# Attention stage: another order of work on PE, VectorE and ScalarE, and three small matrix products in another shape

## The chip, the cores and the metric

The kernel runs on one core of one Trainium2 chip. The metric is the device time of one execution in microseconds (us); lower is better. The profile is of one such execution. PE is TensorE (PEld its weight loads), DVE is VectorE, ACT is ScalarE, POOL is GpSimd, SP issues most of the transfers. A difference of about 0.3% is what the measurement can tell from none.

## The reference, cut to what matters

Pooled attention (8 batches, 8 heads, 576 tokens, 64 columns), a soft mixture of experts whose dispatch weights are a softmax over all tokens, and a dense layer with a gated norm.

```python
k_p = k.reshape(B, H, S // 8, 8, D).mean(axis=3)      # 72 pooled keys
v_p = v.reshape(B, H, S // 8, 8, D).mean(axis=3)
attn = softmax(q @ k_p.T / sqrt(D))                   # 576 x 72 for each head
x = (attn @ v_p) as [B*S, 512]
logits = x @ phi                                      # 32 slots
d = exp(logits - logits.max(0)) / sum over tokens     # dispatch
slot_input = d.T @ x
# ... 8 experts, then c @ slot_out, then the dense layer
```

## The kernel before

The first stage takes the 8 batches one after another. A batch has 5 tiles of tokens: four of 128 tokens and one of 64 (tile 4, in which two groups of heads lie side by side). A batch is written as 5 steps, `t` = 1 to 5, and a step works on several tiles at once: the scores of tile `t + 2`, the sums of tile `t + 1`, the transposes of tile `t`, the logits of tile `t - 1`. Tiles 5, 6 and 7 of a batch are tiles 0, 1 and 2 of the next. Below, 0', 1' and 2' are those tiles of the next batch. The order on each engine is written out by hand, in one `step` function for each engine; batches 1 to 6 run in a loop whose body holds two batches, batch 0 and the end have their own code. There is no scheduler: what is queued behind a wait on its engine waits too.

The path of a tile: `scores` on PE (L1313, tile 4 L1309) writes two PSUM banks of which there is one set. DVE takes the row maximum (L960, `smax`) and subtracts it (L966, into `attn`); only when that is done may `scores` of the next tile start. ACT takes `exps` (L665). DVE sums (L973) and takes the reciprocal (L978), POOL multiplies (L533, `norm`). PE transposes the tile (`aT_t`, L1356, tile 4 L1352), ACT copies the transposes out (`aT_evac`, L641), PE multiplies them by `vphi` (`lt_t`, L1380, tile 4 L1375), ACT copies (`lt_evac`), PE folds the four column groups (`l_t`, L1387), DVE copies the logits (`logit_evac`, L985).

Once a batch:
- `vphi` is pooled v times phi. PE makes `wphi` (`wphi_t`, L1323), ACT copies it out (`wphi_evac`, four copies), PE transposes it (`vphi_t`, L1330 to L1332: three of 128 columns, one of 32 rows, one of 64 rows), DVE copies and folds it (`vphi_evac`, L989 to L991). `lt_t` of tile 0 waits for it.
- the slot maximum of the batch: DVE `lmax_tokens` (L997), PE `lmax_t` (L1396), DVE `new_max` (L1002, then L1006 against the running maximum), PE `mb_t` (L1402, which spreads 32 numbers over 128 partitions with a product over 32 rows), DVE `d_sub` (L1012), ACT `d_exp` (L697, L701), PE `dat_t` (L1416), ACT `dat_evac`, PE `datT_t` (L1425), ACT `datT_evac`, PE `slot_t` (L1434), DVE `slot_acc` (L1022).
- POOL also pools k and v (L374, L378). SP loads k, v and q two batches ahead and an expert's weights in each batch.

`lt_t` has five blocks of the contraction (four of 128 rows, one of 76) and four column groups of 32: blocks 0 to 3 run beside each other in the four groups, block 4 follows alone in group 0.

## Time and profile before

| | us |
|---|---|
| runs shown, median | 441.24 |
| lowest, highest of 3 | 440.08, 441.43 |
| the profiled execution | 440.7 |
| its span | 438.9 |
| scores of batch 1's tile 3 begin | 38.27 |
| the same point of batch 7 | 145.50 |
| first product of the experts | 165.98 |
| dense layer from about | 212 |

Between 38.27 and 145.50 lie six like batches, 17.87 us each. PE's granted clock is full from 19 us on. Of the span PE is busy 94%, DVE 70%, POOL 56%, ACT 54%. A busy PE includes modelled ends of instructions; the distance from one start to the next tells what it really spends. The last 227 us are the dense layer, where PE is busy 221.75 us.

### The profile page before, as it was taken

The page shows a single profiled execution, that of the slowest core. Times are in us where ns is not written, and L with a number is a line of the kernel's source. Part 1 is how long each engine was busy: PE and PEld are TensorE (multiplying, and loading weights), DVE is VectorE, ACT ScalarE, POOL GpSimd, SP SyncE. Part 2 cuts the span into 40 slices and gives each one's busy share as a digit, 9 for nine tenths or more (in the row PEclk, how much of TensorE's full clock was granted, in tenths as well). Part 3 has the DMA queues.
Part 4 walks back from the last instruction along what each step waited for, and adds up shares of the span by engine and source line. Part 5 has one row for each costly group of instructions (what it writes and reads, how often), then busy time and mean ns, then how long its engine had stood idle before and what let it go on. Part 6 is the DMA issues. An engine that isn't in the chain of part 4 may idle for free.

```text
span 438.9 us, 9468 instructions
## 1 busy us (share of the span) xinstructions
PE 413.2 (94%) x3303; PEld 319.1 (73%) x3303; DVE 307.3 (70%) x543; ACT 238.8 (54%) x497; POOL 243.8 (56%) x346
## 2 busy tenths in 40 slices
PE   6788989899899889999899999999999999999997
PEld 6666777677777664455687887888888888888886
DVE  4878788787887747355889976777777777777211
ACT  1457775667756542153777655656555656555310
POOL 2579988888883311020143375757677666676540
PEclk8999999999999999999999999999999999999999
DMA  8847789769695699996001676677666666766732
GB/s 322 331 126 307 309 326 390 288 246 419 247 433 191 231 397 346 431 424 284 1 7 43 131 143 117 130 141 139 134 133 114 135 132 134 143 135 115 157 73 48
DMA packets 79212, 91.68 MB, mean 209 GB/s; under 512 B 67024, under 2 KB 67408, under 8 KB 74448
## 3 DMA queue, kind: packets, MB, share of 16 engines
q1 hardware_dynamic: 74016, 82.07, 60.9%
q10 hardware_dynamic: 5168, 9.24, 6.3%
q8 instruction: 16, 0.26, 0.2%
q14 instruction: 12, 0.10, 0.1%
HBM read 66.13 MB, written 9.44 MB: 172 GB/s over the span
## 4 chain that ended last, share of the span: by engine, by line
PE 75%; DVE 12%; ACT 5%; issue 4%; POOL 3%; DMA 1%; ACTq 0%; DVEq 0%
PE banks L1697 14%; PE banks L1698 14%; PE banks L1699 14%; PE banks L1313 5%; PE banks L1560 3%; PE banks L1669 3%; PE banks L1582 3%; PE banks L1356 2%; PE banks L1416 2%; DVE smax L960 2%; DVE attn L966 2%; DVE ssum L973 2%; PE banks L1387 2%; PE banks L1380 2%; ACT aT L641 1%
## 5 line engine op out<-in xcount | busy, mean ns | idle before, releaser
L1697 PE MATMUL banks<-wo_hi,uh 128*128 128x512 f32 x280 | 110.5, 395 | 0.1
L1698 PE MATMUL banks<-wo_lo,uh 128*128 128x512 f32 x280 | 110.0, 393 | 0.0
L1699 PE MATMUL banks<-wo_hi,ul 128*128 128x512 f32 x280 | 109.1, 390 | 0.0
L609 POOL TENSOR_TENSOR ul<-u_col,uh 128x1024 fp32r<-128x1024 f32 x30 | 71.9, 2397 | 18.6 <-ACT uh L641 18.2
L876 ACT ACTIVATE sq<-u,st 128x1024 f32<-128x1024 f32 x36 | 41.5, 1152 | 39.9 <-DVE u L1198 39.9
L533 POOL TENSOR_TENSOR attn<-attn,srec 128x576 f32<-128x576 f32 (+1 forms) x40 | 43.1, 1078 | 35.5 <-DVE srec L978 35.5
L1697 PEld LDWEIGHTS banks<-wo_hi,uh 128*128 128x128 f32 x280 | 52.6, 188 | 12.7 <-DVE ul L1215 0.5
L1699 PEld LDWEIGHTS banks<-wo_hi,ul 128*128 128x128 f32 x280 | 52.5, 188 | 12.1
L1698 PEld LDWEIGHTS banks<-wo_lo,uh 128*128 128x128 f32 x280 | 52.6, 188 | 11.3
L1198 DVE SCALAR_TENSOR_TENSOR u<-banks,ex 128x1024 f32<-128x1024 f32 x35 | 42.7, 1223 | 24.5 <-ACT ex L867 24.4
L1188 DVE TENSOR_REDUCE st<-banks 128x1 f32<-128x1024 f32 x35 | 42.6, 1216 | 18.3 <-PE banks L1669 18.3
L867 ACT ACTIVATE ex<-banks,st 128x1024 f32<-128x1024 f32 x35 | 39.0, 1115 | 18.4 <-DVE st L1188 17.7
L641 ACT ACTIVATE uh<-u_col 128x1024 fp32r<-128x1024 f32 x30 | 31.7, 1058 | 30.2 <-DMA u_col<-u_blk 16.3
L1313 PE MATMUL banks<-kblk,qb 128*128 128x144 f32 x256 | 40.6, 303 | 5.3 <-DVE attn L966 2.4
L1313 PEld LDWEIGHTS banks<-kblk,qb 128*128 128x128 f32 x256 | 34.0, 194 | 10.1 <-DVE attn L966 4.7
L1229 DVE TENSOR_SCALAR osb<-banks,rs 128x512 f32<-128x512 f32 x35 | 25.9, 741 | 19.5 <-PE banks L1699 19.5
L665 ACT ACTIVATE attn<-attn 128x576 f32<-128x576 f32 (+1 forms) x40 | 25.4, 636 | 25.5 <-DVE attn L966 25.1
L1208 DVE STREAM_TRANSPOSE u_blk<-u 128x1024 f32<-128x1024 f32 x30 | 37.4, 1246 | 1.9
L595 POOL TENSOR_SCALAR st<-st 128x1 f32<-128x1 f32 x36 | 6.9, 191 | 52.5 <-ACT sq L876 52.2
L374 POOL TENSOR_TENSOR vraw<-vraw 128x1152 f32<-128x1152 f32 (+1 forms) x14 | 29.5, 2108 | 7.4 <-DMA vraw<-in_v 7.4
L960 DVE TENSOR_REDUCE smax<-banks 128x8 f32<-128x576 f32 (+1 forms) x40 | 27.2, 680 | 8.4 <-PE banks L1313 8.4
L973 DVE TENSOR_REDUCE ssum<-attn 128x8 f32<-128x584 f32 (+1 forms) x40 | 27.8, 694 | 6.7 <-ACT attn L665 6.4
(179 smaller groups left out, 692.0 us busy)
## 6 DMA issues: line engine op xcount, KB each, us to landing
...
```

The lines of the kernel that those rows point to most:

```text
L533: pool.tensor_tensor(a, a, per_head(srec[bit(tile)], t)[:, :, :, None].to_broadcast([P, tile_pairs(t), 2, SP]), ALU.mult) \
L609: pool.tensor_tensor(ul[par][:, :, :].rearrange("p c (q t) -> p (c q) t", q=4), v, uh[par][:, :, :].bitcast(F32).rearrange("p c (q t) -> p ...
L867: act.activation(ex[par][:, :, :], h_banks(par), ACT.Exp, bias=st[k % STATS]["nmax"][:, :], accum_out=st[k % STATS]["den"][:, :]).then_inc ...
L876: act.activation(sq[par][:, :], u[k % URING][:, :], ACT.Square, scale=-float(FF), bias=st[k % STATS]["usum"][:, :], accum_out=st[k % STATS ...
L973: dve.tensor_reduce(per_head(ssum[par], t), head_sums(tile[1], t), AX.X, ALU.add).then_inc(sem("ssum"), 1)
L1188: dve.tensor_reduce(st[k % STATS]["nmax"][:, :], h_banks(k % 2), AX.XY, ALU.max, negate=True).then_inc(sem("nmax"), 1)
L1198: dve.scalar_tensor_tensor(u[k % URING][:, :].rearrange("p (a n) -> p a n", a=2), h_banks(par), 1.0, ex[par][:, :, :], ALU.mult, ALU.mult, ...
L1208: dve.transpose(u_blk[slot][:, :, :, k % 2, :].rearrange("p c q t -> p (c q) t"), u[k % URING][:, :].rearrange("p (b f) -> p b f", f=BLK)) \
L1313: last = pe.matmul(s_view[:, j, 0:2 * SP], q_cols(par, t, j), kblk[par][:, j, :], start=True, stop=True)
L1697: pe.matmul(ps[4 + par], uh[par][:, c, :], wo_hi[:, c, :], start=(c == 0), stop=False)
L1698: pe.matmul(ps[4 + par], uh[par][:, c, :], wo_lo[:, c, :], start=False, stop=False)
L1699: last = pe.matmul(ps[4 + par], ul[par][:, c, :], wo_hi[:, c, :], start=False, stop=(c == FC - 1))
```

## The change

It has two parts.

*Shapes.* `vphi_t` becomes four transposes of 128 rows; `wphi` is 512 columns wide, and its last 76 columns lie in partitions where the fourth block leaves room, so ACT copies five pieces. In `lt_t` the fifth block, of 76 rows, is no longer one product of 128 columns in group 0 but four of 32 columns, one in each group (tile 4: four of 32 columns in place of two of 64). `mb_t` takes all 128 rows; DVE's running maximum becomes a `tensor_scalar` with the old maximum as a pointer scalar.

*Order.* On PE, DVE and ACT the steps of batches 1 to 7 are written out anew. POOL and SP keep their order. Batch 0 keeps its order but for `vphi_evac` of batch 1, which stands at its end; `lmax_tokens` and the last `logit_evac` of a batch move into step 1 of the next.

```diff
-        wphi = bump("wphi", [P, PAIRS * PAIR])
+        wphi = bump("wphi", [P, 4 * P])
...
                 for j in range(PAIRS):
-                    g = 32 * GROUP[j]
-                    last = copy(wphi[g:g + 32, PAIR * j:PAIR * (j + 1)], b_head[g:g + 32, 0:PAIR])
-                last.then_inc(sem("wphi_sb"), 1)
+                    g, n = 32 * GROUP[j], min(PAIR, 4 * P - PAIR * j)
+                    copy(wphi[g:g + 32, PAIR * j:PAIR * j + n], b_head[g:g + 32, 0:n])
+                copy(wphi[LAST_ROWS, 0:BLOCKS[4]], b_head[LAST_ROWS, PAIR - BLOCKS[4]:PAIR]).then_inc(sem("wphi_sb"), 1)
...
+                elif t == 1:
+                    aT_evac(ahead(b, par, 0), 0)
+                    aT_evac(ahead(b, par, 0), 1)
+                    lt_evac(ahead(b, par, 0))
+                    aT_evac(ahead(b, par, 1), 0)
+                    aT_evac(ahead(b, par, 1), 1)
+                    if not last:
+                        kblk_fill(b + 1, 1 - par, 0)
+                    exps(ahead(b, par, 3))
+                    if last:
+                        v72_evac(b, par)
+                    else:
+                        kblk_fill(b + 1, 1 - par, 1)
+                elif t == 2:
+                    lt_evac(ahead(b, par, 1))
+                    exps(ahead(b, par, 4))
+                    aT_evac(ahead(b, par, 2), 0)
+                    d_exp(b - 1, (False,))
+                    v72_evac(b, par)
+                    aT_evac(ahead(b, par, 2), 1)
+                    vpad_fill(b + 1, 1 - par)
+                elif t == 3:
+                    lt_evac(ahead(b, par, 2))
+                    d_exp(b - 1, (True,))
+                    exps(ahead(b, par, 5))
+                    aT_evac(ahead(b, par, 3), 0)
+                    aT_evac(ahead(b, par, 3), 1)
                     alpha_exp(b - 1, 1 - par)
+                    dat_evac(b - 1)
+                elif t == 4:
+                    lt_evac(ahead(b, par, 3))
+                    aT_evac(ahead(b, par, 4), 0)
+                    aT_evac(ahead(b, par, 4), 1)
+                    exps(ahead(b, par, 6))
+                    datT_evac(b - 1)
+                    wphi_evac(b + 1)
+                else:
+                    lt_evac(ahead(b, par, 4))
+                    exps(ahead(b, par, 7))
...
-                dve.tensor_tensor(slot_max[par][:, :], lmax_new[:, :], slot_max[1 - par][:, :], ALU.max).then_inc(sem("m_ready"), 1)
+                dve.tensor_scalar(slot_max[par][:, :], lmax_new[:, :], slot_max[1 - par][:, :], None, ALU.max).then_inc(sem("m_ready"), 1)
...
+                    logit_evac(ahead(b, par, -1))
+                    tile_sums(ahead(b, par, 2))
+                    lmax_tokens(b - 1)
+                    tile_max(ahead(b, par, 3))
+                    tile_rec(ahead(b, par, 2))
+                    tile_sub(ahead(b, par, 3))
+                    batch_max(b - 1)
+                    logit_evac(ahead(b, par, 0))
+                    running_max(b - 1, 1 - par)
+                elif t == 2:
+                    sub_max(ahead(b, par, 4))
+                    d_sub(b - 1)
+                    tile_sums(ahead(b, par, 3))
+                    tile_rec(ahead(b, par, 3))
+                    logit_evac(ahead(b, par, 1))
+                    tile_sums(ahead(b, par, 4))
+                elif t == 3:
+                    tile_max(ahead(b, par, 5))
+                    tile_rec(ahead(b, par, 4))
+                    tile_sub(ahead(b, par, 5), dat_count(b - 1, 0))
+                    tile_sums(ahead(b, par, 5))
+                    logit_evac(ahead(b, par, 2))
+                    tile_rec(ahead(b, par, 5))
+                elif t == 4:
+                    tile_max(ahead(b, par, 6))
                     den_acc(b - 1, 1 - par)
-                if not (last and t + 2 >= TILES) and not (first and t in (1, 3)):
-                    sub_max(ahead(b, par, t + 2), None if t != 3 or first else dat_count(b - 1, 0))
-                if not first:
-                    if t == 1:
-                        new_max(b - 1, 1 - par)
-                    if t == 2:
-                        d_sub(b - 1)
-                    if t == 5:
-                        slot_acc(b - 1, 1 - par)
-                logit_evac(ahead(b, par, t - 1))
-                if t == 5:
-                    lmax_tokens(b)
+                    tile_sub(ahead(b, par, 6))
+                    logit_evac(ahead(b, par, 3))
+                    tile_sums(ahead(b, par, 6))
+                else:
+                    tile_max(ahead(b, par, 7))
+                    tile_rec(ahead(b, par, 6))
+                    tile_sub(ahead(b, par, 7))
+                    slot_acc(b - 1, 1 - par)
+                    vphi_evac(b + 1, 1 - par)
...
-                for n in range(1, 4):
-                    pe.transpose(b_head[:, 32 + P * (n - 1):32 + P * n], wphi[:, P * n:P * (n + 1)], ident[:, :])
-                pe.transpose(b_head[:, 0:32], wphi[0:32, 0:P], ident[0:32, 0:32])
-                pe.transpose(b_head[0:BLOCKS[4], 32 + 3 * P:96 + 3 * P], wphi[0:64, 4 * P:4 * P + BLOCKS[4]], ident[0:64, 0:64]).then_inc(sem("vphi_ps"), 1)
+                for n in range(4):
+                    last = pe.transpose(b_head[:, P * n:P * (n + 1)], wphi[:, P * n:P * (n + 1)], ident[:, :])
+                last.then_inc(sem("vphi_ps"), 1)
...
-                    for k, m in enumerate(BLOCKS):
-                        g = k % 4
-                        last = pe.matmul(b_lt[32 * g:32 * (g + 1), 0:P], vphi[par][0:m, k, :], aT[bit(tile)][0:m, k, :],
-                                         start=(k < 4), stop=(k + 4 >= NB), tile_position=(0, 32 * g))
+                    for k in range(4):
+                        pe.matmul(b_lt[32 * k:32 * (k + 1), 0:P], vphi[par][:, k, :], aT[bit(tile)][:, k, :],
+                                  start=True, stop=False, tile_position=(0, 32 * k))
+                    for g in range(4):
+                        r = slice(32 * g, 32 * (g + 1))
+                        last = pe.matmul(b_lt[r, r], vphi[par][0:m, NB - 1, :], aT[bit(tile)][0:m, NB - 1, r], start=False, stop=True, tile_position=(0, 32 * g))
...
-                pe.matmul(bank[:, 0:SLOTS], slot_max[par][0:SLOTS, :].to_broadcast([SLOTS, P]), ident[0:SLOTS, 0:SLOTS], start=True, stop=True).then_inc(sem("mb_ps"), 1)
+                pe.matmul(bank[:, 0:SLOTS], slot_max[par][:, :].to_broadcast([P, P]), ident[:, 0:SLOTS], start=True, stop=True).then_inc(sem("mb_ps"), 1)
...
+                    scores(ahead(b, par, 3))
+                    lt_t(ahead(b, par, 0))
+                    aT_t(ahead(b, par, 1))
+                    l_t(ahead(b, par, 0))
+                    lmax_t(b - 1, 1 - par)
+                elif t == 2:
+                    scores(ahead(b, par, 4))
+                    lt_t(ahead(b, par, 1))
+                    mb_t(b - 1, 1 - par)
+                    aT_t(ahead(b, par, 2))
+                    l_t(ahead(b, par, 1))
+                elif t == 3:
+                    scores(ahead(b, par, 5))
+                    dat_t(b - 1, 1 - par, (0, 1))
+                    lt_t(ahead(b, par, 2))
+                    dat_t(b - 1, 1 - par, (2, 3))
+                    l_t(ahead(b, par, 2))
+                    aT_t(ahead(b, par, 3))
+                elif t == 4:
+                    scores(ahead(b, par, 6))
+                    dat_t(b - 1, 1 - par, (4,))
+                    lt_t(ahead(b, par, 3))
+                    aT_t(ahead(b, par, 4))
+                    datT_t(b - 1)
+                    wphi_t(b + 1)
+                    l_t(ahead(b, par, 3))
+                else:
+                    scores(ahead(b, par, 7))
+                    slot_t(b - 1, 1 - par)
+                    v72_t(b + 1, 1 - par)
+                    lt_t(ahead(b, par, 4))
+                    vphi_t(b + 1)
+                    l_t(ahead(b, par, 4))
+                    aT_t(ahead(b, par, 5))
```

DVE, from the end of step 5 into step 1 of the loop's second batch. `smax` is the maximum, `attn` the subtraction, `ssum` and `srec` sum and reciprocal, `c_all` a tile's logits, `lmax_new` and `slot_max` the slot maximum. Before:

```order
L966 TENSOR_TENSOR attn<-banks,smax_86 128x4x2x72
L1022 SCALAR_TENSOR_TENSOR acc_slot<-acc_slot,alpha_94,banks 128x128
L985 ISA
L985 COPY c_all<-banks 128x32
L997 TENSOR_REDUCE lmax<-c_all 128x32
L988 REGISTER_ALU
L989 COPY vphi_80<-banks 128x32
L990 TENSOR_REDUCE vphi_80<-banks 128x96
L991 COPY vphi_80<-banks 76x32
L973 TENSOR_REDUCE ssum_88<-attn 128x8
L978 RECIPROCAL srec_90<-ssum_88 128x8
L959 REGISTER_ALU
```

and after:

```order
L989 TENSOR_TENSOR attn<-banks,smax_86 128x4x2x72
L1054 SCALAR_TENSOR_TENSOR acc_slot<-acc_slot,alpha_94,banks 128x128
L1019 REGISTER_ALU
L1020 COPY vphi_80<-banks 128x32
L1021 TENSOR_REDUCE vphi_80<-banks 128x96
L1022 COPY vphi_80<-banks 76x32
L1016 ISA
L1016 COPY c_all<-banks 128x32
L998 TENSOR_REDUCE ssum_88<-attn 128x8
L1028 TENSOR_REDUCE lmax<-c_all 128x32
L981 REGISTER_ALU
L982 TENSOR_REDUCE smax_87<-banks 128x8
```

`vphi_evac` has moved ahead of the logits of the old batch, `lmax` behind the sums of tile 2, and the reciprocal of tile 2 behind the maximum of tile 3.

ACT, step 1 of the same batch (`aT` the transposes, `lt` the product's copy, `attn` the exponential). Before:

```order
L641 ACTIVATE lt_68<-banks 128x128
L664 REGISTER_ALU
L665 ACTIVATE attn<-attn 128x4x2x72
L675 ISA
L641 ACTIVATE aT_79<-banks 128x512
L675 REGISTER_ALU
L641 ACTIVATE aT_79<-banks 76x128
L641 ACTIVATE kblk_75<-kp 64x4x72
```

and after:

```order
L642 ACTIVATE lt_68<-banks 128x128
L676 ISA
L642 ACTIVATE aT_79<-banks 128x512
L676 REGISTER_ALU
L642 ACTIVATE aT_79<-banks 76x128
L646 REGISTER_ALU
L642 ACTIVATE kblk_75<-kp 64x4x72
L665 REGISTER_ALU
L666 ACTIVATE attn<-attn 128x4x2x72
```

The exponential of tile 3 stands behind the copies of tile 1's transposes, no longer ahead of them.

PE, step 5 of the loop's first batch (L1313/L1377 scores of 2', L1434/L1503 `slot_t`, L1375/L1438 and L1442 `lt_t` of tile 4, L1356/L1419 `aT_t` of 0', L1387/L1456 `l_t`, L1340/L1403 `v72_t`, L1330/L1394 `vphi_t`). Before:

```order
L1313 MATMUL banks<-kblk_67,qb_62 128x144 x4
L1434 MATMUL banks<-v_0_82,datT 32x64 x8
L1364 ISA
L1375 MATMUL banks<-aT_79,vphi_81 32x64 x6
L1356 MATMUL banks<-ident,attn 128x128 x4
L1356 MATMUL banks<-ident,attn 76x128
L1387 MATMUL banks<-fold_50,lt_69 128x32
L1340 MATMUL banks<-ident,vT_76 72x128 x4
L1330 MATMUL banks<-ident,wphi 128x128 x3
L1331 MATMUL banks<-ident,wphi 128x32
L1332 MATMUL banks<-ident,wphi 76x64
```

and after:

```order
L1377 MATMUL banks<-kblk_67,qb_62 128x144 x4
L1503 MATMUL banks<-v_0_82,datT 32x64 x8
L1403 MATMUL banks<-ident,vT_76 72x128 x4
L1427 ISA
L1438 MATMUL banks<-aT_79,vphi_81 32x64 x4
L1442 MATMUL banks<-aT_79,vphi_81 32x32 x4
L1394 MATMUL banks<-ident,wphi 128x128 x4
L1456 MATMUL banks<-fold_50,lt_69 128x32
L1419 MATMUL banks<-ident,attn 128x128 x4
L1419 MATMUL banks<-ident,attn 76x128
```

`v72_t` and `vphi_t` have moved up, `l_t` of tile 4 and `aT_t` of tile 0' to the end.

## Rows read from the trace of the kernel before

**Rows 1.** Busy time by engine in one batch: stretch, length, busy (instructions), clock, DMA.
```profile
73.75:91.78 18.03, 16.64 (x214) 13.10 (x213) 14.53 (x34) 12.12 (x36) 14.77 (x12) 1.00 0.82 321
```

**Rows 2.** Waits of two batches (73.75 to 109.61): total us, times, longest.
```profile
PE banks L1380 <- ACT aT L641: 1.3, 2, 0.7
...
PEld banks L1387 <- ACT lt L641: 1.3, 6, 0.3
```

**Rows 3.** Timeline, scores of tile 3 in batches 1 and 7: start, length, what.
```profile
38.27 1.25 PE L1313 MATMUL banks<-kblk,qb 128*128 128x144 f32 x8
...
145.50 1.25 PE L1313 MATMUL banks<-kblk,qb 128*128 128x144 f32 x8
```

**Rows 4.** Timeline of PE over batch 3, without weight loads.
```profile
73.76 1.25 PE L1313 MATMUL banks<-kblk,qb 128*128 128x144 f32 x8
74.94 0.42 PE L1396 MATMUL banks<-ident,lmax 128*32 128x128 f32 x8
75.18 0.60 PE L1380 MATMUL banks<-aT,vphi 128*32 128x128 f32 x10
...
77.11 0.71 PE L1309 MATMUL banks<-kblk,qb 128*64 128x144 f32 x8 [0.49 <-DVE attn L966]
78.47 0.63 PE L1380 MATMUL banks<-aT,vphi 128*32 128x128 f32 x10 [0.65 <-ACT aT L641]
79.03 0.40 PE L1402 MATMUL banks<-ident,slot_max 32*128 32x32 f32 x2
79.36 0.77 PE L1356 MATMUL banks<-ident,attn 128*128 128x128 f32 x5
...
80.50 1.24 PE L1313 MATMUL banks<-kblk,qb 128*128 128x144 f32 x8 [0.22 <-issue]
...
84.67 1.25 PE L1313 MATMUL banks<-kblk,qb 128*128 128x144 f32 x8
...
87.79 1.25 PE L1313 MATMUL banks<-kblk,qb 128*128 128x144 f32 x8
88.98 0.43 PE L1434 MATMUL banks<-v,datT 72*32 72x64 f32 x16
89.25 0.42 PE L1375 MATMUL banks<-aT,vphi 128*32 128x64 f32 x12
...
90.57 0.61 PE L1340 MATMUL banks<-ident,vT 128*72 128x128 f32 x4
91.01 0.49 PE L1330 MATMUL banks<-ident,wphi 128*128 128x128 f32 x3
...
91.79 1.25 PE L1313 MATMUL banks<-kblk,qb 128*128 128x144 f32 x8
```

**Rows 5.** Timeline of DVE, POOL and ACT in step 1 of the same batch.
```profile
75.52 0.74 DVE L960 TENSOR_REDUCE smax<-banks 128x8 f32<-128x576 f32 x1
...
76.30 0.76 DVE L966 TENSOR_TENSOR attn<-banks,smax 128x576 f32<-128x576 f32 x1
...
76.79 1.41 POOL L374 TENSOR_TENSOR vraw<-vraw 128x576 f32<-128x576 f32 x1
...
77.09 0.68 ACT L665 ACTIVATE attn<-attn 128x576 f32<-128x576 f32 x1 [1.00 <-DVE attn L966]
...
77.29 0.93 DVE L1006 TENSOR_TENSOR slot_max<-lmax_new,slot_max 128x1 f32<-128x1 f32 x1
77.68 0.74 ACT L641 ACTIVATE aT<-banks 128x512 f32<-128x512 f32 x2
```

**Rows 6.** One line, all its instructions: ns min/median/max; then a row of the timeline.
```profile
L1006 DVE TENSOR_TENSOR slot_max<-lmax_new,slot_max x8: 158/929/942, 41.8 to 159.2; 128x1 f32<-128x1 f32 x8
...
90.62 0.34 DVE L1022 SCALAR_TENSOR_TENSOR acc_slot<-acc_slot,alpha,banks 128x128 f32<-128x128 f32 x1
```

**Rows 7.** Groups of two batches: busy us, mean ns of one.
```profile
L641 ACT ACTIVATE wphi<-banks 32x147 f32<-32x147 f32 x8 | 2.2, 280 | 0.1
```

**Rows 8.** Busy time from the end of the attention stage into the experts, columns as in rows 1.
```profile
146.00:206.00 60.00, 56.91 (x716) 31.16 (x714) 33.98 (x78) 22.57 (x53) 9.85 (x16) 1.00 0.97 385
```

181 lines of the change are left out of this document (84 added, 97 removed).

## The prediction, made before the changed kernel had run

> **What bounds the kernel now.** I read the table of busy time by stretch first. In a batch of the loop no engine but PE is near its limit: of 18.03 us PE is busy 16.64, POOL 14.77, DVE 14.53, ACT 12.12 [rows 1]. POOL and DVE are close enough behind that PE can't fall far before one of them takes over. The loop takes (145.50 - 38.27) / 6 = 17.87 us a batch [rows 3], all of it at PE's full clock.
>
> Then the waits and the timeline of PE. Twice in each batch PE stands still on the tile chain: 0.49 us before the scores of tile 4, which wait for DVE's subtraction of tile 3, and 0.65 us before `lt_t` of tile 1, which waits for ACT's copy of the transposes [rows 2, 4]. Three times `l_t` waits for ACT's `lt_evac`, 1.3 us in six waits of two batches, so 0.22 each [rows 2]. And 0.22 us before the scores of 0' is issue [rows 4]. That is 0.49 + 0.65 + 3 x 0.22 + 0.22 = 2.0 us of standing still in a batch, and 16.0 us of work.
>
> The scores have one set of banks, so a second limit is the chain scores, maximum, subtraction: 1.25 + 0.74 + 0.76 = 2.75 us and some hand-over for each full tile [rows 4, 5]. Four of these and a short one are near 13 us: not the bound by itself, but it decides wherever DVE or PE starts its part late.
>
> **The change, part by part.** I cut a batch at the starts of scores on PE: 3 to 4 is 77.11 - 73.76 = 3.35 us, 4 to 0' is 80.50 - 77.11 = 3.39, 0' to 2' is 87.79 - 80.50 = 7.29, 2' to the next 3 is 91.79 - 87.79 = 4.00, together 18.03 [rows 4].
>
> *Price of the new `lt_t`.* Now its start and the next start are 79.03 - 78.47 = 0.56 apart [rows 4]. A round of four products of 128 columns side by side takes 75.18 - 74.94 = 0.24, so the lone fifth with the turn-over costs 0.32. Eight products of 64 columns take 89.25 - 88.98 = 0.27, four of them 0.14 [rows 4]; four of 32 columns are between half of that and all of it, 0.07 to 0.14. They replace a lone stream of 128 columns, for which the round of 0.24 is the nearest row: gain 0.10 to 0.17. I take 0.12 for each full tile, nothing for tile 4. The bound below nothing: if the four short products don't overlap, each at 0.06 (0.24 / 4), the round costs 0.24 and the gain is nil; with a fresh turn-over besides it may lose 0.1.
>
> *Price of `vphi_t`.* Now 91.79 - 91.01 = 0.78, of which the two pieces of other row counts are the second half; four transposes of `v72_t` take 91.01 - 90.57 = 0.44 [rows 4]. Gain 0.34. *`mb_t`* takes 79.36 - 79.03 = 0.33 with a change of the row shape ahead of it and behind it [rows 4]; on all rows one of these goes: gain 0.13, taken as 0.2 for the product that is left.
>
> *3 to 4.* DVE sets this. Now the maximum starts 75.52 - 73.76 = 1.76 us after the scores [rows 5], since `vphi_evac` and the sums of tile 2 stand in front. The change sends `vphi_evac` ahead into the time in which PE does `v72_t`, `vphi_t` and `aT_t`, but puts `lmax` in front (it stood behind tile 4's logits), and the reciprocal of tile 2 between maximum and subtraction. I lay DVE out from its subtraction of 2', which ends about 0.5 us before the scores of 3: slot sum, `vphi_evac`, logits, sums and `lmax` carry it to +1.55; maximum, reciprocal, subtraction to +3.2. PE needs only about 2.6 us in that time. 3.35 becomes 3.25: the stall before tile 4 stays, in the main.
>
> *4 to 0'.* The 0.65 us wait goes: the copies of tile 1's transposes stand ahead of the exponential of tile 3 on ACT, and that exponential had run from 77.09 with the copies at 77.68 [rows 5]. Of `lt_t` 0.12 and of `mb_t` 0.13 go too. 3.39 - 0.65 - 0.25 = 2.49. What is queued behind the exponential that now comes later is the sum of tile 3 on DVE and its norm on POOL; the transposes of tile 3 come over 3 us later, which hides it. The issue gap of 0.22 stays: the same four waits stand there.
>
> *0' to 2'.* Products of `dat_t` and `l_t` change places, which costs nothing by itself. Two `lt_t` give 0.24, and two of the three waits for `lt_evac` go, since each `l_t` now has another product in front: 0.38, rather than 0.44, as I leave some for the left copy behind `vpad_fill`. 7.29 - 0.62 = 6.67.
>
> *2' to 3.* `vphi_t` gives 0.34, the third wait 0.22: 4.00 - 0.56 = 3.44.
>
> Sum: 3.25 + 2.49 + 6.67 + 3.44 = 15.85 us. This supposes that every hand-over works at once, and three have no slack: DVE's sums of 1' now stand ahead of the maximum of 2' and end as those scores do; `vphi_t` waits for five copies of 0.28 us [rows 7] behind an exponential that used to stand behind them, and now gates `l_t` and `aT_t`; `m_ready` comes as `mb_t` is due. I add 0.25, about one tenth of a microsecond for each: 16.1 us a batch. POOL, with 14.77 us of work in 16.1 [rows 1], still fits, and so does DVE.
>
> Over six batches: 6 x (17.87 - 16.1) = 10.6 us. Batch 0 keeps its order and has five `lt_t` and two `vphi_t`; most of it waits for POOL and DVE, so of 4 x 0.12 + 2 x 0.34 = 1.2 I take 0.5. In batch 7 the wait of 0.65 goes and some of the shapes count: 0.8.
>
> *What is behind it.* From 146 to 206 the DMA engines are busy 97% [rows 8]: the experts' weights arrive just as they are used, so whatever the end of the attention gains beyond the start of these transfers is lost. That start hangs on `vphi_t` of batch 7, which moves up by `l_t` and `aT_t`, some 0.8 us. So the 0.8 may pass, no more, and zero is its lower bound. The gain in batches 1 to 6 passes whole, since the transfers begin earlier by as much. The dense layer doesn't change.
>
> Total: 10.6 + 0.5 + 0.8 = 11.9 us. The profiled execution took 440.7 us (span 438.9); 440.7 - 11.9 = 428.8 us. The median of the runs shown is 0.5 us above it, which is inside their spread.
>
> **The rivals.**
>
> *The running maximum still waits for POOL.* L1006 handles one number per partition, and took 0.158 us at its shortest and 0.929 at the median [rows 6]. In the timeline it starts at 77.29 and ends at 78.22, when POOL's addition ends, 76.79 + 1.41 = 78.20 [rows 5]: it has two inputs in SBUF, and stands still while POOL adds. The change makes the second a pointer scalar. L1022, with a tensor and a pointer scalar in SBUF and its third input in PSUM, runs 0.34 us beside a POOL addition [rows 6]; from that I take it that the wait goes. But L1022 is not a `tensor_scalar`. If the wait stays, it now falls in front of the maximum of tile 4 on DVE and ahead of `mb_t` on PE, with up to 1.4 us of POOL's addition still to run: about 0.9 us a batch, 5.4 in all, 434.2 us. For: POOL will be busier. Chance 0.15.
> The Trainium skill, "SBUF — State Buffer", section "Who interferes with whom", names `tensor_scalar` among the operations that can use both port pairs and then contend with GpSimd, when its operands meet a condition on even sizes; one number per partition is at its edge. By that rule it would be this rival, 434.2 us; the rows of before have no such instruction beside a busy POOL, so none settles it.
>
> *The short products are bound by their weight loads.* Then `lt_t` gets slower by 0.1 instead of faster by 0.12: 4 x 0.22 = 0.9 us a batch, 434.2 us too. Against: eight products take 0.27 with eight loads [rows 4]. Chance 0.08.
>
> *PE and nothing else.* If DVE is early enough that the stall before tile 4 goes as well (0.5 us) and the 0.25 isn't needed, a batch takes 15.4 us: 424.6 us. Against: DVE's own 3.2 us. Chance 0.12.
>
> *Half of the stalls come back elsewhere* (ACT's `vpad_fill`, which now stands earlier and waits for POOL, holds `lt_evac` and the exponential of 0'): some 1.2 us a batch more, 436 us. Chance 0.08.
>
> *Slower.* The ring through ACT: scores of 1', maximum, subtraction, exponential, `datT` copy, five `wphi` copies, `vphi_t`, `l_t`, `aT_t`, scores of 3. Its parts to the last copy are 1.25 + 0.74 + 0.76 + 0.68 and 5 x 0.28 = 4.8 us [rows 4, 5, 7], and with the rest it is level with PE's own way. Each microsecond by which ACT or DVE is late there adds one to the batch, because the next scores are queued behind. It turns the sign when it is late by 2.0 us (11.9 / 6); at 2.5 us late the time is 444 us. Nothing in the rows makes it that late. Chance 0.05.
>
> *Nothing gained.* The waits are only renamed, as PE is 94% busy on the page: 440.7. Against: the distances of starts show 2 us of standing still. Chance 0.04.
>
> **How the numbers follow.** The forecast, 428.8, has 0.48. The range runs from 424.5 to 436.0: it holds the forecast with both bounds of `lt_t`, the two rivals at 434.2 and most of the one at 424.6, 0.8 in all. Faster by over 0.3%: 0.48 + 0.15 + 0.08 + 0.12 + 0.08 = 0.91. Within 0.3%, about what a measurement of this kernel can tell from no change: 0.04. Slower: 0.05.
>
> **What would show it.** Right: starts of the scores of tile 3 about 16.1 us apart; from scores of 4 to those of 0' near 2.5 us with no wait before `lt_t`; `lt_t` to the next start 0.44, `vphi_t` 0.44; `slot_max` at 0.16 us in all batches; a stall of about half a microsecond still in front of tile 4. Wrong: `slot_max` near 0.9 us; `vphi_t` waiting for ACT's copies or `aT_t` for POOL; or weights that land late, with PE waiting for DMA after the attention.

## The result and the profile after

The changed kernel takes 425.38 us (median of 4, 425.07 to 426.57), the kernel before 440.66 in the same comparison (median of 4, 439.25 to 441.43): ratio 0.9662, 95% interval 0.9628 to 0.9695. The profiled execution took 425.07 us, with a span of 423.3 in place of 438.9. The forecast was 428.8, the range 424.5 to 436.0.

Busy time by engine in batch 3 of the changed kernel, columns as in [rows 1]; then the scores of tile 3 in batches 1, 3 and 7 on the timeline of PE (start, length, what), which answer to [rows 3]:

```profile
68.65:84.20 15.55, 15.28 (x242) 12.65 (x241) 13.14 (x36) 12.30 (x36) 14.71 (x12) 1.00 0.91 373
```

```profile
36.59 0.29 PE L1377 MATMUL banks<-kblk,qb 128*128 128x144 f32 x1
...
68.65 0.29 PE L1377 MATMUL banks<-kblk,qb 128*128 128x144 f32 x1
...
130.41 0.29 PE L1377 MATMUL banks<-kblk,qb 128*128 128x144 f32 x1
```

(130.41 - 36.59) / 6 = 15.64 us a batch in place of 17.87: 16.68 for batch 1, 15.43 for the other five. Batch 1 is longer because batch 0 keeps its old order: VectorE stands idle 0.75 us for `vphi_t`, takes it only at 36.79, behind the start of the scores, and PE waits 0.63 us before the scores of tile 4. POOL has the same work as in [rows 1] and is now busy 14.71 of 15.55 us, so nearest to its limit behind PE; whether it comes next no run shows. The span splits like this:

| stretch | before | after | difference | forecast |
|---|---|---|---|---|
| start to scores of batch 1's tile 3 | 38.27 | 36.59 | -1.68 | -0.5 |
| six batches | 107.23 | 93.82 | -13.41 | -10.6 |
| to the first product of the experts | 20.48 | 21.06 | +0.58 | -0.8 |
| experts and dense layer | 272.92 | 271.83 | -1.09 | 0 |
| span | 438.9 | 423.3 | -15.6 | -11.9 |

PE over batch 3 of the changed kernel, the same places as in [rows 4]:

```profile
68.65 1.15 PE L1377 MATMUL banks<-kblk,qb 128*128 128x144 f32 x8
69.73 0.43 PE L1446 MATMUL banks<-aT,vphi 128*32 128x128 f32 x8
69.97 0.26 PE L1450 MATMUL banks<-aT,vphi 76*32 76x32 f32 x8
70.16 0.77 PE L1419 MATMUL banks<-ident,attn 128*128 128x128 f32 x5
...
71.43 0.71 PE L1373 MATMUL banks<-kblk,qb 128*64 128x144 f32 x8
72.08 0.42 PE L1446 MATMUL banks<-aT,vphi 128*32 128x128 f32 x8
72.32 0.24 PE L1450 MATMUL banks<-aT,vphi 76*32 76x32 f32 x8
72.49 0.41 PE L1471 MATMUL banks<-ident,slot_max 128*128 128x32 f32 x2
72.74 0.74 PE L1419 MATMUL banks<-ident,attn 128*128 128x128 f32 x5
...
73.82 1.24 PE L1377 MATMUL banks<-kblk,qb 128*128 128x144 f32 x8
...
79.57 0.38 PE L1494 MATMUL banks<-ident,dat 128*72 128x128 f32 x2 [0.18 <-DVE acc_den L1049]
...
80.52 1.23 PE L1377 MATMUL banks<-kblk,qb 128*128 128x144 f32 x8
...
82.91 0.66 PE L1394 MATMUL banks<-ident,wphi 128*128 128x128 f32 x4
83.40 0.38 PE L1456 MATMUL banks<-fold,lt 128*128 128x32 f32 x2
```

Both stalls of [rows 4], 0.49 before the scores of tile 4 and 0.65 before `lt_t`, are gone, and so is the 0.22 of issue before the scores of 0', which the prediction had left standing. What PE still waits for in two batches (68.65 to 99.58; total us, times, longest), where [rows 2] had 1.3 us for the copies of the transposes and 1.3 in six waits of weight loads (PEld) for `lt`:

```profile
PEld banks L1456 <- ACT lt L642: 0.5, 2, 0.3
...
PE banks L1494 <- DVE acc_den L1049: 0.4, 2, 0.2
```

And the running maximum, all its instructions as in [rows 6] (ns min/median/max):

```profile
L1038 DVE TENSOR_SCALAR slot_max<-lmax_new,slot_max x8: 214/215/215, 40.3 to 142.8; 128x1 f32<-128x1 f32 x8
```

The three shapes: `lt_t` takes 70.16 - 69.73 = 0.43 to the next start (before 0.56), `mb_t` 0.25 (0.33), `vphi_t` 0.49 (0.78).

The experiments are read by one measure that the rest of the span doesn't disturb: the four stretches of a batch between starts of scores on PE, as in the prediction, here as means over the six batches that follow the scores of batch 1's tile 3. Each row is read from that kernel's profile.

| kernel | 3 to 4 | 4 to 0' | 0' to 2' | 2' to 3 | batch |
|---|---|---|---|---|---|
| before | 3.31 | 3.23 | 7.33 | 4.00 | 17.87 |
| max_only | 3.31 | 3.00 | 7.23 | 3.99 | 17.53 |
| shapes_only | 3.41 | 2.87 | 7.24 | 3.81 | 17.33 |
| order_only | 2.94 | 2.33 | 6.80 | 4.08 | 16.14 |
| after | 2.92 | 2.30 | 6.73 | 3.68 | 15.64 |
| max_two_tensors | 2.92 | 2.30 | 6.74 | 3.68 | 15.64 |
| old_lt | 2.95 | 2.37 | 6.80 | 3.70 | 15.82 |
| exp_first | 2.92 | 2.79 | 6.71 | 3.69 | 16.12 |
| vphi_late | 3.18 | 2.15 | 6.77 | 3.68 | 15.78 |
| pe_old_order | 3.64 | 2.67 | 6.83 | 3.40 | 16.54 |
| kblk_early | 2.92 | 2.13 | 6.77 | 3.68 | 15.50 |
| combined | 2.92 | 2.06 | 6.75 | 3.68 | 15.41 |

### The profile page after: what moved, and what is told of

It is laid out like the page before. It is cut to its first block, busy times and chain, and to the rows that moved or that the text cites. A ratio compares the mean times of both kernels' runs of the same rounds, so it can differ in the third digit from the quotient of the medians.

```text
span 423.3 us, 9911 instructions
## 1 busy us (share of the span) xinstructions
PE 403.5 (95%) x3519; PEld 315.7 (75%) x3519; DVE 299.6 (71%) x543; ACT 240.7 (57%) x505; POOL 243.6 (58%) x346
## 4 chain that ended last, share of the span: by engine, by line
PE 73%; DVE 8%; ACT 7%; issue 5%; POOL 4%; DMA 2%; ACTq 0%; POOLq 0%; DVEq 0%
PE banks L1784 15%; PE banks L1783 14%; PE banks L1785 14%; PE banks L1377 4%; PE banks L1646 3%; PE banks L1755 3%; PE banks L1668 3%; PE banks L1419 2%; ACT attn L666 2%; DVE smax L982 2%; DMA wo_raw<-in_moe_w_out 2%; POOL kraw L375 1%; POOL attn L534 1%; DVE st L1252 1%; PE banks L1456 1%
## 5 line engine op out<-in xcount | busy, mean ns | idle before, releaser
L534 POOL TENSOR_TENSOR attn<-attn,srec 128x576 f32<-128x576 f32 (+1 forms) x40 | 43.0, 1077 | 18.7 <-DVE srec L1005 18.3
L1377 PE MATMUL banks<-kblk,qb 128*128 128x144 f32 x256 | 38.2, 292 | 3.9 <-DVE attn L989 2.8
L1377 PEld LDWEIGHTS banks<-kblk,qb 128*128 128x128 f32 x256 | 33.1, 190 | 5.6 <-DVE attn L989 4.0
L642 ACT ACTIVATE aT<-banks 128x512 f32<-128x512 f32 (+1 forms) x80 | 29.0, 407 | 9.4 <-PE banks L1419 8.3
```

Of the source, the lines that this page charges most:

```text
L534: pool.tensor_tensor(a, a, per_head(srec[bit(tile)], t)[:, :, :, None].to_broadcast([P, tile_pairs(t), 2, SP]), ALU.mult) \
L642: return act.activation(o, i, ACT.Copy, scale=scale)
L1377: last = pe.matmul(s_view[:, j, 0:2 * SP], q_cols(par, t, j), kblk[par][:, j, :], start=True, stop=True)
```

## The experiments

### Shapes against order

`shapes_only` is the kernel before with the new `wphi`, `vphi_t`, `lt_t`, `mb_t` and the new running maximum; `order_only` is the changed kernel with the old `wphi`, `vphi_t`, `lt_t` and `mb_t`.

> The kernel before in its old order, with the new shapes alone (four whole transposes for vphi_t, fifth block of lt_t over four groups, mb_t over all rows, running maximum with a pointer scalar). Theory (shapes and order add up): the trace of the changed kernel shows lt_t 0.43 us instead of 0.56, vphi_t 0.49 instead of 0.78, mb_t 0.25 instead of 0.33. Of these the lt_t of tile 0 lies in the stretch that waits for VectorE and gives nothing; 3 x 0.13 + 0.29 + 0.08 = 0.76 us a batch, 4.6 us in six batches, and about 0.5 elsewhere: 435.5 us against 440.7. The 0.49 and 0.65 us stalls of PE stay. Rival (the old order is bound by the chain through VectorE and ACT, PE's gains turn into waits): under 2 us gained, 439 or more, and the two stalls longer than before.

> The changed kernel with the old shapes of vphi_t (and its copies), lt_t and mb_t; the new order and the one-operand running maximum stay. Theory (shapes and order add up): each lt_t costs 0.13 us more, now all four of a batch are on PE's own path, vphi_t 0.29, mb_t 0.08: 0.89 us a batch, 5.3 in six batches, 0.5 elsewhere: 425.4 + 5.8 = 431.2 us. Rival (order does all of it, since PE had slack once the stalls are gone): under 428 us.

Measured: `shapes_only` 436.71 us (ratio to before 0.9905, 0.9871 to 0.994) and 17.33 a batch; `order_only` 430.29 us (0.9744, 0.9699 to 0.9789) and 16.14 a batch. In the loop 17.87 - 17.33 = 0.54 and 17.87 - 16.14 = 1.73 make 2.27, where the changed kernel gained 2.23, but that is no proof that the parts add up: both kernels have the new running maximum, which alone is worth 0.34 in the old order (`max_only`, below). Without it the three products' shapes gave 17.53 - 17.33 = 0.20 in the old order and 16.14 - 15.64 = 0.50 in the new one, for 0.76 and 0.89 expected. So the order, with the new maximum, is three quarters of the gain, and the shapes are worth more than twice as much in the new order as in the old. Of their 0.50 the stretch with `vphi_t` has 0.40. The rival was right for one stretch: in the old order, what PE saves between the scores of 3 and 4 turns into waiting. PE in `shapes_only`:

```profile
71.41 1.15 PE L1314 MATMUL banks<-kblk,qb 128*128 128x144 f32 x8
...
74.85 0.71 PE L1310 MATMUL banks<-kblk,qb 128*64 128x144 f32 x8 [0.83 <-DVE attn L967]
76.22 0.43 PE L1383 MATMUL banks<-aT,vphi 128*32 128x128 f32 x8 [0.65 <-ACT aT L642]
```

The stall of 0.49 has become 0.83, and the distance to tile 4 has not become shorter (3.31 before, 3.41 here). The stall of 0.65 is as it was.

### One shape, put back

```diff
-                    for k in range(4):
-                        pe.matmul(b_lt[32 * k:32 * (k + 1), 0:P], vphi[par][:, k, :], aT[bit(tile)][:, k, :],
-                                  start=True, stop=False, tile_position=(0, 32 * k))
-                    for g in range(4):
-                        r = slice(32 * g, 32 * (g + 1))
-                        last = pe.matmul(b_lt[r, r], vphi[par][0:m, NB - 1, :], aT[bit(tile)][0:m, NB - 1, r], start=False, stop=True, tile_position=(0, 32 * g))
+                    for k, m in enumerate(BLOCKS):
+                        g = k % 4
+                        last = pe.matmul(b_lt[32 * g:32 * (g + 1), 0:P], vphi[par][0:m, k, :], aT[bit(tile)][0:m, k, :],
+                                         start=(k < 4), stop=(k + 4 >= NB), tile_position=(0, 32 * g))
...
```

The lines for tile 4, put back likewise, are left out here.

> The changed kernel with one shape put back: in lt_t the fifth block is again one product of 128 columns in group 0 (tile 4: two of 64). The traces of the two kernels that have the new order show lt_t 0.54 against 0.43 us, but of the four stretches of a batch only the one with vphi_t got much shorter by the shapes (4.08 to 3.68); the others 2.83 to 2.78, 2.36 to 2.39, 6.80 to 6.70. Theory (in the new order most of what lt_t gains is waited away before the next scores and before datT_t): 0.15 us a batch longer at most, up to 1 us in all, 425.4 to 426.4 us. Rival (the price by the piece holds): 4 x 0.12 = 0.48 a batch, 2.9 in six, 428.3 us.

Measured: 427.15 us (0.9691, 0.9656 to 0.9726), 15.82 a batch against 15.64. Four `lt_t` that are each 0.11 longer (0.54 to the next start) cost 0.18 together, a little above the theory and far from 0.48. What the shorter `lt_t` gains is waited away again in most places: from 3 to 4 the scores wait for VectorE's chain, from 4 to 0' `l_t` waits for ACT (below), and `datT_t` now waits 0.18 for `acc_den`, in the row at 79.57 above.

### The form of the running maximum

```diff
-                dve.tensor_scalar(slot_max[par][:, :], lmax_new[:, :], slot_max[1 - par][:, :], None, ALU.max).then_inc(sem("m_ready"), 1)
+                dve.tensor_tensor(slot_max[par][:, :], lmax_new[:, :], slot_max[1 - par][:, :], ALU.max).then_inc(sem("m_ready"), 1)
```

in the changed kernel (`max_two_tensors`), and the opposite edit alone in the kernel before (`max_only`).

> The changed kernel with one instruction put back: the running maximum of the slots as an operation with two tensor inputs in SBUF. Theory (it was this form that stood still while POOL adds, and the new one does not): it takes near 0.9 us again in most batches, where the changed kernel shows 0.21, and since it now stands ahead of the maximum of tile 4 on VectorE and of mb_t on PE, it costs 0.3 to 0.7 us a batch: 427.5 to 430 us. Rival (what made it fast is its new place, not its form): 0.2 us in the trace and 425.4 us. Second rival: 0.9 us in the trace, but covered, 425.4 us.

> The kernel before, with one instruction changed: the running maximum with a pointer scalar in place of a second tensor. Put back into the changed kernel it cost nothing, since there it falls at the end of a POOL instruction and took 0.23 to 0.28 us; in the old order it begins in the middle of POOL's addition and took 0.93. Theory (in the old order the 0.7 us that it blocks VectorE lies ahead of the maximum of tile 4 and lengthens the stretch from tile 4 to 0' a little): 0.21 us in the trace and 0.1 to 0.3 us a batch, 0.6 to 1.8 us in all, 439 to 440.3. Rival (PE waits for ACT's copy there anyway): nothing, 441 us. Second rival (the short form too stands still in the old place): 0.93 in the trace.

Measured: `max_two_tensors` 426.33 us (0.966, 0.9618 to 0.9703), the loop unchanged at 15.64; the theory of 0.3 to 0.7 a batch fell, and the first rival was right. `max_only` 439.07 us (0.9975, 0.9956 to 0.9995), 17.53 a batch, 0.34 less than before, above what was expected; the wait lay on the path from 4 to 0'. The total moved by 0.8 us only, but between executions of like mean granted clock (last section) the spans differ by 1.9 to 2.6 us, which fits six times 0.34. DVE and POOL in `max_only`, then in `max_two_tensors`, both beside a working POOL:

```profile
75.07 1.41 POOL L374 TENSOR_TENSOR vraw<-vraw 128x576 f32<-128x576 f32 x1
...
75.56 0.21 DVE L1006 TENSOR_SCALAR slot_max<-lmax_new,slot_max 128x1 f32<-128x1 f32 x1
```

```profile
87.61 1.15 POOL L534 TENSOR_TENSOR attn<-attn,srec 128x576 f32<-128x576 f32 x1
...
88.54 0.24 DVE L1038 TENSOR_TENSOR slot_max<-lmax_new,slot_max 128x1 f32<-128x1 f32 x1
```

At the same place in the order as [rows 5], inside POOL's addition, the form with a pointer scalar takes 0.21 us and the one with two tensors 0.93. That settles the form. In the new order the instruction with two tensors starts at 88.54 and ends at 88.78, 0.02 us behind POOL's product (87.61 + 1.15 = 88.76), as the one in [rows 5] ends 0.02 behind POOL's addition: it still waits, but only the rest. In other batches it ends in the same way at 42.00 and 73.28, where POOL ends at 41.98 and 73.26. So either the form or the new place would have done, and the two gains don't add. The Trainium skill, "SBUF — State Buffer", section "Who interferes with whom", says that an instruction of VectorE with two inputs in SBUF contends with a GpSimd instruction that reads SBUF, and calls the shared ports an exclusive lock for whoever issues first. The 0.93 us, which end with the addition that had begun before, agree. Its warning on `tensor_scalar` did not apply to this one, by the 0.21 us.

### ACT: exponential or copies first

```diff
+                    exps(ahead(b, par, 3))
                     aT_evac(ahead(b, par, 1), 0)
                     aT_evac(ahead(b, par, 1), 1)
                     if not last:
                         kblk_fill(b + 1, 1 - par, 0)
-                    exps(ahead(b, par, 3))
```

> The changed kernel with ACT's exponential of tile 3 again ahead of the copies of tile 1's transposes, in every batch of the loop; nothing else. Theory (this one exchange made the 0.65 us stall before lt_t of tile 1 and its removal): the copies come 0.7 us later, PE waits 0.6 to 0.8 us before lt_t of tile 1 again, and of that 0.5 or more lasts: 3 to 4.5 us in all, 428.5 to 430 us. Rival (the stretch is set by another queue, and the exponential's earlier place gives back as much by earlier sums of tile 3): 425.4 us within 0.7.

Measured: 428.55 us (0.9705, 0.9676 to 0.9734), 16.12 a batch, so 0.48 more, all of it from 4 to 0' (2.30 to 2.79). PE in `exp_first`:

```profile
75.59 0.42 PE L1446 MATMUL banks<-aT,vphi 128*32 128x128 f32 x8 [0.65 <-ACT aT L642]
```

It is the wait of [rows 4] again, to the hundredth. The exchange on ACT is what removed it. Of 0.65 us only 0.48 are the batch's: `l_t` of tile 1 no longer waits behind ACT's other work, and from its start to the scores of 0' it is 0.24 us (76.83 to 77.07) where the changed kernel has 0.49 (73.33 to 73.82).

### VectorE: when vphi is taken

```diff
...
                 elif t == 1:
                     logit_evac(ahead(b, par, -1))
+                    vphi_evac(b, par)
...
                     slot_acc(b - 1, 1 - par)
-                    vphi_evac(b + 1, 1 - par)
```

> The changed kernel with VectorE's three instructions for vphi back in step 1 of the batch, behind the logits of the old batch and ahead of the sums of tile 2, as before the change. In the changed kernel they run in the 0.9 us before the scores of tile 3 end, so the order of the queue is the same but for one copy of 0.1 us. Theory (the stall before tile 4 went because VectorE reaches the maximum of tile 3 just as the scores end, whatever stands in what order ahead of it): nothing changes, 425.4 us within 0.5. Rival (the early vphi is what removed it, since lt_t of tile 0 waits for it): lt_t of tile 0 and the maximum of tile 3 come later, 0.3 us a batch, 427 us or more.

Measured: 426.43 us (0.9658, 0.963 to 0.9686), which the total alone doesn't tell from the changed kernel; in the profile 15.78 a batch, 3 to 4 longer by 0.26 and 4 to 0' shorter by 0.15. My theory fell; the rival's 0.3 came from 3 to 4 in the main, and half of it was won back behind it, for a reason that no run here isolates. DVE in `vphi_late`, whose scores of tile 3 begin at 70.22:

```profile
69.27 0.34 DVE L1054 SCALAR_TENSOR_TENSOR acc_slot<-acc_slot,alpha,banks 128x128 f32<-128x128 f32 x1
69.97 0.19 DVE L1016 COPY c_all<-banks 128x32 f32 x1 [0.36 <-PE banks L1454]
70.08 0.19 DVE L1020 COPY vphi<-banks 128x32 f32<-128x32 f32 x1
...
71.76 0.75 DVE L982 TENSOR_REDUCE smax<-banks 128x8 f32<-128x576 f32 x1
```

The logits of the old batch's tile 4 come late from PE (`l_t` stands behind `vphi_t` there). With `vphi_evac` ahead of them DVE fills that time; behind them it stands idle 0.36 us, and its maximum of tile 3 starts 71.76 - 70.22 = 1.54 us after the scores, where the changed kernel has 69.83 - 68.65 = 1.18, which is when the scores end.

### PE's own order

The five steps of PE in the loop in their old order, VectorE and ACT new.

> The changed kernel with the loop's five steps on PE in the old order (lmax_t ahead of lt_t, l_t straight behind aT_t, datT_t behind l_t, v72_t and vphi_t at the end); VectorE, ACT and all shapes stay new. The new order as a whole gave 1.73 us a batch (17.87 to 16.14, old shapes), of which ACT's exchange is 0.48 and VectorE's place for vphi 0.15. Theory (most of the remaining 1.1 us is PE's own order, which puts another product between lt_t and l_t and between the copies and vphi_t): 15.64 becomes 16.5 to 16.8 a batch, 431 to 432.5 us, with waits of l_t for ACT's lt again. Rival (VectorE's queue brought it): under 16.0 a batch, 427.5 us or less.

Measured: 431.84 us (0.9806, 0.9766 to 0.9847), 16.54 a batch. The size is as expected, the reason mostly another. PE in `pe_old_order`:

```profile
73.09 0.43 PE L1465 MATMUL banks<-ident,lmax 128*32 128x128 f32 x8 [0.95 <-DVE lmax L1028]
...
77.00 0.41 PE L1456 MATMUL banks<-fold,lt 128*128 128x32 f32 x2 [0.26 <-ACT lt L642]
```

PE's old place for `lmax_t`, right behind the scores, meets VectorE's new, later place for `lmax`: 0.95 us of waiting that neither kernel has. `l_t` waits for ACT as expected, but 0.26. From 2' to 3 the old order on PE is even faster (3.40 against 3.68). So the orders of the engines are one table: the 0.90 us is no price of PE's part alone, and how the remaining 1.1 us of the order divide over the engines stays open.

### Behind the loop

```diff
             col_sum(0)
-            pe.wait_ge(sem("wo_in1"), 32)
-            col_sum(1).then_inc(sem("col_ps"), 1)
             for tiles in ((0, 1), (2, 3), (4,)):
                 dat_t(B - 1, 1, tiles)
-            keep_clock(ps[5], 4)
+            pe.wait_ge(sem("wo_in1"), 32)
+            col_sum(1).then_inc(sem("col_ps"), 1)
```

> The changed kernel, with the second half of the column sums of the output weights on PE behind the last batch's dispatch products, in place of the four filler products there: PE no longer stands 1.45 us before them for the transfer of those weights. Theory (the experts' stage goes at the pace of the weights' transfers, so what is gained ahead of it is lost in it): 425.4 us within 0.5, the first product of the experts earlier, the stage longer by as much. Rival (the end of the attention is the path): up to 1.4 us less, 424.0 us.

Measured: 425.4 us (0.963, 0.9583 to 0.9677). From the scores of batch 7's tile 3 (130.79) to the first product of the experts (151.10) it is 20.31 us, 0.75 less than in the changed kernel. The experts did not take it back: from the first product of the first expert to that of the last it is 32.85 or 32.86 us in all fourteen profiles, however early or late they begin, and 16.55 to 16.57 from there to the dense layer; in none of them does PE stand still for 0.15 us or more between the experts' products. So the theory fell. In this profile's total two other things hide the gain: the dense layer, unchanged code that took 222.4 to 223.5 us in the fourteen profiles (223.2 in this one, 222.4 in the changed kernel's) and not longer for beginning earlier, and 0.35 us ahead of batch 1's tile 3, where the two have the same code. In the ratios the intervals of the two kernels overlap.

What the edit took off the path is another transfer, that of the output weights. The weight load of the second half of the column sums, in the changed kernel:

```profile
145.06 0.20 PEld L1591 LDWEIGHTS banks<-wo_raw,gT 128*32 128x32 f32 x8 [1.45 <-DMA wo_raw<-in_moe_w_out]
```

In the kernel before this wait of a weight load is 0.71 us, and PE's own products don't stand still for it. In seven of the eleven profiles with the new order they do, for 0.20 to 1.27 us. So the prediction's rule holds here, for another transfer than the one it named (the numbers are in the part on the prediction).

### A better place for the key blocks' copy

ACT in the changed kernel, from tile 4 to 0':

```profile
72.53 0.44 ACT L642 ACTIVATE kblk<-kp 64x288 f32<-64x288 f32 x1
73.00 0.28 ACT L642 ACTIVATE lt<-banks 128x128 f32<-128x128 f32 x1
```

`lt_t` of tile 1 ends at about 72.5, its copy runs from 73.00, and `l_t`, behind which the scores of 0' are queued, needs it. The edit moves half of the key blocks' copy into a time in which ACT stands idle:

```diff
+                    if not last:
+                        kblk_fill(b + 1, 1 - par, 0)
                     lt_evac(ahead(b, par, 0))
                     aT_evac(ahead(b, par, 1), 0)
                     aT_evac(ahead(b, par, 1), 1)
-                    if not last:
-                        kblk_fill(b + 1, 1 - par, 0)
                     exps(ahead(b, par, 3))
```

> The changed kernel with ACT's first half of the key blocks' copy (0.33 us) moved from between the copies of tile 1's transposes and the exponential of tile 3 to where ACT stands idle 0.79 us before lt_evac of tile 0. In the changed kernel lt_evac of tile 1 runs 0.5 us after its product, behind the second half of that copy, and l_t of tile 1 and the scores of the next batch's tile 0 wait for it. Theory (from tile 4 to tile 0' ACT's queue is now the bound, which is why the shorter lt_t and mb_t gave nothing there): 2.39 becomes 2.15, 0.24 us a batch, 1.4 us in all, 424.0 us. Rival (issue and the scores' own chain set it): 425.4 us within 0.4.

Measured: 423.81 us (0.9602, 0.9576 to 0.9628), 15.50 a batch: 4 to 0' is 2.13 in place of 2.30. 0.14 a batch, 0.8 in six, where 0.24 and 1.4 were expected: I had read the stretch in a batch with 2.39, and every second one had 2.17 already. The mechanism was right. The total moved by 1.6 us; what goes beyond the loop's 0.8 is no gain of the edit, as three of these four executions had a mean clock of 0.998 to 0.999 and the changed kernel's four 0.991 to 0.996.

### Fillers, and all of it together

> The changed kernel with more filler transposes on PE where it stands idle outside the loop: ten more ahead of the first scores, three ahead of lmax_t of batch 7 and four ahead of mb_t of batch 7. Across the ten profiles so far PE's granted clock is half for some 3 us in one of two places: behind the first scores (4 of 10, where PE had been idle 1.9 to 2.4 us) or in the column sums of the tail (4 of 10), and each fall costs 1.0 to 1.3 us of the span. Theory (the idle time ahead brings the fall): no fall at either place, the runs closer together, 424.3 us. Rival (the fall comes whatever PE does there): falls as often as before, 425.4 us.

> The changed kernel with everything that the runs point to: the first half of the key blocks' copy early on ACT (15.50 us a batch in place of 15.64), the second half of the column sums behind the dispatch products, the last batch's logits of tile 1 on VectorE ahead of the subtraction of tile 4 (PE waits 0.87 us for them), and the fillers. The experts took 32.86 us in all ten profiles, so gains ahead of them should pass. Theory: 0.8 from the loop, 0.9 from the tail, 0.6 from fewer falls of the clock against the changed kernel's 425.4: 423.1 us. Rival (the tail's gains are lost to transfers after all): 424 us.

Measured: `fillers` 424.95 us (0.9644, 0.961 to 0.9678), three of its four executions at a mean granted clock of 1.000 and one at 0.996, spans 422.5 to 423.5. As a time the total doesn't tell it from the changed kernel, and `kblk_early` has 0.998 to 0.999 in three of four executions without any filler. `combined` 423.38 us (0.9595, 0.9561 to 0.9628), with 15.41 a batch and 16.0 us from the scores of batch 7's tile 4 to the experts, where the changed kernel has 18.3 and `kblk_early`, without a fall of the clock there, 16.95: 0.9 for the two edits of the tail and the fillers together, as expected, though the wait for the output weights differs from profile to profile too. Its spans are 420.0 to 422.3, with a mean clock of 0.992 in three of five executions: the fall of the clock was not prevented, it came elsewhere (last section). It is the fastest kernel here, but against `kblk_early` (423.81) the intervals can't tell it from no change.

## Why the prediction was right, and where its steps were off

The direction and the range held, and so did the account of the 0.65 us wait. The size was 3.4 us short, and the time lies 0.9 us inside the lower end of the range: the rival "PE and nothing else" (15.4 us a batch, 424.6 us, chance 0.12) is what happened, with 15.43 in five of the six batches. The sign "a stall of about half a microsecond still in front of tile 4" came in batch 1 alone, and one of the signs of being wrong, PE waiting for a transfer at the end of the attention, did come.

*3 to 4, forecast 3.25, measured 2.79 in the like batches.* This step was furthest off: it kept a stall that went. DVE in the changed kernel:

```profile
67.02 0.76 DVE L989 TENSOR_TENSOR attn<-banks,smax 128x576 f32<-128x576 f32 x1
67.69 0.34 DVE L1054 SCALAR_TENSOR_TENSOR acc_slot<-acc_slot,alpha,banks 128x128 f32<-128x128 f32 x1
68.05 0.19 DVE L1020 COPY vphi<-banks 128x32 f32<-128x32 f32 x1
68.15 0.55 DVE L1021 TENSOR_REDUCE vphi<-banks 128x96 f32<-128x384 f32 x1
68.62 0.18 DVE L1022 COPY vphi<-banks 76x32 f32<-76x32 f32 x1
68.72 0.18 DVE L1016 COPY c_all<-banks 128x32 f32 x1
68.81 0.75 DVE L998 TENSOR_REDUCE ssum<-attn 128x8 f32<-128x584 f32 x1
69.48 0.42 DVE L1028 TENSOR_REDUCE lmax<-c_all 128x32 f32 x1
69.83 0.76 DVE L982 TENSOR_REDUCE smax<-banks 128x8 f32<-128x576 f32 x1
70.50 0.19 DVE L1005 RECIPROCAL srec<-ssum 128x8 f32<-128x8 f32 x1
70.62 0.76 DVE L989 TENSOR_TENSOR attn<-banks,smax 128x576 f32<-128x576 f32 x1
```

The subtraction of 2' ends at 67.02 + 0.76 = 67.78, and from there to the maximum it is 69.83 - 67.78 = 2.05 us, exactly what the forecast had (from -0.5 to +1.55). What was wrong is where it began: the subtraction ended 0.87 us before the scores (68.65), not 0.5. Of these 0.37 us PE brought 0.24, since its stretch from 2' to 3 took 3.68 and not 3.44, and the chain of scores, maximum and subtraction of 2' the rest. Another 0.10 came behind, from the maximum to the end of the subtraction (1.55 for 1.65). With that the maximum begins as the scores end, the bare chain is left, 2.79 us, and `vphi_late` shows how little slack there was. So the errors of this stretch and of the one before it are one error in part: what PE lost there gave VectorE its lead here.

*4 to 0', forecast 2.49, measured 2.24 in the like batches.* The 0.65 us wait went, and for the reason given (`exp_first`). The forecast began from batch 3's 3.39, where the mean of the six is 3.23: the 0.22 of issue stands in two of the six batches only, and in none after. The same 0.16 a batch is short in the sum, since 16.1, built from a batch of 18.03, was taken from the mean of 17.87. Not seen was that the running maximum also lay on this stretch: `max_only` shows 0.24 here and 0.10 in the next. The prediction had it as a danger of the new order only; as that it did not come, 0.21 us in each batch (forecast 0.16). And of the shapes' 0.25 next to nothing arrived here (2.33 to 2.30): ACT's copy of the key blocks held `l_t`, and moving half of it away brought 0.17 (`kblk_early`).

*0' to 2', forecast 6.67, measured 6.72. 2' to 3, forecast 3.44, measured 3.68.* `vphi_t` went from 0.78 to 0.49, not 0.44, and the third wait of 0.22 was exchanged for a place that is no better: with PE's old order and the new shapes the stretch takes 3.40. That wait was also read too high. [rows 2] gives it for the weight loads, which overlap PE's products; on PE itself no `l_t` of the six batches before stood still for more than 0.07 us, and from `aT_t` to `l_t` it is 0.72 us at two of the places (82.73 to 83.45, 89.60 to 90.32) where it is 0.61 without the wait (79.36 to 79.97). So these waits cost PE about 0.1 each, and the 2.0 us of standing still in the prediction are some 0.4 too many.

*The shapes* were priced right by the piece (`lt_t` 0.43 for a forecast 0.44, `vphi_t` 0.49 for 0.44, `mb_t` 0.25 for 0.2) and counted wrongly. The four stretches hold 3 x 0.12 + 0.34 + 0.13 = 0.83 us a batch of them; they gave 0.50 in the new order (16.14 to 15.64), and in the old one 0.20 (17.53 to 17.33), the maximum left out. *The order*, with the new maximum, was to give the rest, 1.77 - 0.83 = 0.94, and gave 1.73. Two errors of opposite sign, 0.33 too much and 0.79 too little, make a forecast that looks better than its parts; in that much it was luck.

*The 0.25 for hand-overs* wasn't needed in the like batches.

*Ahead of the loop and behind it*, most of the surprise is the granted clock and a transfer, not the change. PE's clock is in the column before the last two. Before, behind the first scores; after, in the column sums; then `kblk_early`, which has the changed kernel's code there:

```profile
10.00:12.00 2.00, 2.00 (x11) 1.99 (x11) 1.04 (x2) 0.00 (x0) 1.60 (x1) 0.50 1.04 389
```

```profile
144.00:146.00 2.00, 1.87 (x16) 0.28 (x12) 1.54 (x2) 0.87 (x4) 0.00 (x0) 0.50 1.09 455
```

```profile
144.00:146.00 2.00, 1.65 (x16) 0.29 (x12) 1.85 (x3) 0.95 (x4) 0.00 (x0) 1.00 1.08 450
```

0.50 is the level of 1.2 GHz, 1.00 that of 2.4. The first scores took 2.26 us in the profile of before and 1.22 in that of after, code that the change doesn't touch; `max_only`, without that fall, has old shapes and order and starts batch 1's tile 3 at 36.95, where the changed kernel has 36.59 and `tail_split`, the same code up to there, 36.94. So 1.3 of the 1.68 us is chance and 0 to 0.4 the change, for a forecast of 0.5. Behind the loop the table shows 0.58 us more where 0.8 less was forecast. From the second half of the column sums to the experts' first product the changed kernel takes 6.41 us, at the lower clock in part, where `kblk_early` has 5.28 and the kernel before 5.25: that fall hid 1.1. What lies ahead of it depends on the transfer of the output weights, for which PE waits in `kblk_early` and `max_two_tensors`, both without a fall there:

```profile
145.18 1.06 PE L1591 MATMUL banks<-wo_raw,gT 128*32 128x512 f32 x8 [0.35 <-DMA wo_raw<-in_moe_w_out]
```

```profile
146.93 1.06 PE L1591 MATMUL banks<-wo_raw,gT 128*32 128x512 f32 x8 [1.27 <-DMA wo_raw<-in_moe_w_out]
```

From the scores of batch 7's tile 3 to the first column sum both have gained what the changed kernel has, 1.29 and 1.35 us (13.05 and 12.99, before 14.34). At the second half, behind that wait, `kblk_early` has 0.77 left (14.46, before 15.23) and `max_two_tensors` nothing (15.33), and to the experts it is 19.74 and 20.59 us, before 20.48. So the forecast's 0.8 is met in one profile and missed whole in the other: what passes there is set by when the transfer lands. The 1.09 us less in experts and dense layer is the dense layer's own spread.

*What the prediction said would hold back the end* (97% busy transfers, [rows 8]) was for the experts a share of busy time taken for a bound: their stage has one length whenever it begins. The transfer that did hold PE was that of the output weights ahead of them; of the 1.3 us gained up to there it kept 0.5 in one profile and all in another.

The gain as a whole does not hang on where the clock fell: in executions of a mean clock of 0.995 to 0.996 the spans average 438.9 us before (6 of them) and 423.6 after (2), at 0.991 to 0.992 440.1 (13) and 424.1 (2).
